# A fused attention, mixture and channel-mixing kernel on one core: buffers that TensorE reads start at multiples of 128 bytes

## Chip, cores and metric

One core of a Trainium2 chip. The metric is the device time of one execution in microseconds (us). The kernel before takes 463.05 us, the median of 3 runs (462.33 to 463.84).

## The reference

Three layers over 2 sequences of 768 tokens with 512 features, all in float32:

```python
# 1. attention, 8 heads of 64: local band (96 back) and 8 global keys, with a slope per head
a = softmax(scale * q @ k.T + bias, masked);  x = a @ v              # (2, 768, 512)
# 2. four causal attention experts, the best two of each token weighted by a gate
logits = x @ w_gate                                                   # (512, 4)
for e in range(4):
    q, k, v = x @ wq[e], x @ wk[e], x @ wv[e]                         # (512, 64) each
    out += weight[e] * (softmax(scale * q @ k.T, causal) @ v @ wo[e])
# 3. token mixing of rank 32, then a channel MLP with a hidden size of 2048
u = out + U/V mixed out
return u + relu(u @ w_ch1) @ w_ch2
```

## The kernel before

**Two forms of a product.** Layer 1 and the attention matrices of layer 2 are plain float32 matmuls. Every product with a weight matrix is made of float32r matmuls: `split_product` (line 1212) takes each operand as a high part and a low part (names ending in h and l) and issues high by high, high by low and low by high into the same PSUM tile. All of its matmuls carry line 1218 in the profile. One operand is the stationary one (loaded by a weight load, 128 columns), the other is the moving one, streamed past it.

```python
for wh, wl, mh, ml in groups:
    for a, m in ((wh, mh), (wh, ml), (wl, mh)):
        last = pe.matmul(dst, a, m, start=start and k == 0, stop=stop and k == n - 1, **kw)
```

**Who uses it.**
- `projected` (line 1274): queries and keys of the experts. Stationary: `wqk_h`, `wqk_l`. Moving: 512 or 256 columns of `xh`, `xl`, the split output of layer 1.
- `values_of` (line 1330): values and gate logits. Stationary: 128 columns of `xh`, `xl`. Moving: a row of 260 columns of `wv_h`, `wv_l` (256 of wv, 4 of w_gate), 12 such matmuls for each of 12 tiles.
- `both_weights` (line 1344): the product of wo and w_ch1, in 8 pieces of 256 columns, 24 matmuls each. Stationary: `woT_h`, `woT_l`. Moving: a piece of w_ch1, which lies in a part of `xh`, `xl` that is free by then (6 pieces), or in `wqk_h`, `wqk_l` (pieces 5 and 6, after the projections are done with them).
- `whole` (line 1558), once for each sequence: u itself. Stationary: `wo_h`, `wo_l`. Moving: the mixed tokens, which lie in `xh[:, 1]`, `xl[:, 1]`.
- `hidden` and `second` (lines 1572 and 1588): the MLP, 32 steps f (16 for each sequence). `hidden(f)` is 12 matmuls, 6 with 512 and 6 with 256 moving columns of `xh`, `xl` against `w01_soon` or `w01_late`. `second(f)` is 24 matmuls, 12 with 512 and 12 with 256 columns of `hidh`, `hidl` against `fh`, `fl`; it reads the same buffers for both sequences.

By these loops there are 720 such matmuls with 512 moving columns (384 in `second`, 192 in `hidden`, 96 in `projected`, 48 in `whole`), 912 with 256 (384, 192, 96, 48, and 192 in `both_weights`) and 144 with 260, 1776 in all.

**The other matmuls.** Transposes (lines 1250, 1383, 1465, 1493) have `prob`, `prob_2`, `o32` as stationary and `ident` as moving operand. Scores (1237, 1449), attention by values (1270, 1482) and the rank product of `nat` by `umix` (1394) are float32 and run in two passes each.

**Order.** Each engine has its own instruction list, written out by hand, with semaphores between them. TensorE's list runs attention with the first projections woven in (from about 0 to 94 us), then the experts' attention with the weight products put between as a filling (list `FILL`, to 238 us), then `whole`, and from 252 us the MLP: `hidden(f+1)` ahead of `second(f)`. In the MLP ScalarE writes `hidh` (line 792), VectorE writes `hidl` (1201) and `fh` (1162), GpSimd writes `fl` (492), and SyncE loads `fraw`. GpSimd also splits the value weights, one row of 260 columns at a time, in `split_weight` (line 504), from `wraw` into `wv_h` and `wv_l`.

**Where buffers begin.** `sb` (line 134) places buffers on each of the 128 partitions one behind the other, each rounded up to 32 bytes. `ident` begins at byte 16512, a multiple of 128. `tie` takes 64 bytes behind it, so what follows begins 64 bytes past a multiple of 128, until `wgt` (192 bytes) ends that; `wv_h` (4 rows of 1040 bytes) and the gate buffers bring it back. For the kernel before this gives:

| begins | buffers that TensorE reads |
|---|---|
| at a multiple of 128 | `ident`, `wqk_h`, `wqk_l`, `wv_h`, `woT_h`, `woT_l`, `wo_h`, `wo_l`, `fh`, `fl`, `w01_soon`, `w01_late`, `mq`, `mk`, `mv`, `prob_2`, `qT`, `kT`, `vN`, `vB` |
| 64 past one | `xh`, `xl`, `prob`, `probT`, `hidh`, `hidl`, `wv_l`, `o32`, `nat`, `umix`, `vmix`, `t3` |

The slices that matmuls take of them begin at further multiples of 128 bytes, but for the value weights: their four rows begin 0, 16, 32 and 48 bytes past a multiple of 128 in `wv_h`, and 64, 80, 96 and 112 in `wv_l`.

Of the kernel before, what the change touches and what calls it, by code (L numbers as in the profile page):

```python
# [15 lines left out]
F32R = mybir.dt.float32r  # L16
# [5 lines left out]
P = 128  # L22
# [6 lines left out]
KT = DM // P  # L29
# [101 lines left out]
def build(nc, t, out):  # L131
    ctx = ExitStack()
    with ctx:
        def sb(name, shape, dt=F32, where=ctx):
            return where.enter_context(nc.sbuf_tensor(name, shape, dt))
# [12 lines left out]

        ident = sb("ident", [P, P])
        tie = sb("tie", [P, E, E])  # L150
        xh = sb("xh", [P, B, KT, S], F32R)
        xl = sb("xl", [P, B, KT, S], F32R)
        prob = sb("prob", [P, 4, S])
# [10 lines left out]
        seps = sb("seps", [P, 2 * (N_UNIT + M_UNIT)])  # L164
        sinv = sb("sinv", [P, 2 * (N_UNIT + M_UNIT)])
        wgt = sb("wgt", [P, 2 * M_UNIT])

        wqk_h = sb("wqk_h", [P, KT, 512], F32R)
        wqk_l = sb("wqk_l", [P, KT, 512], F32R)
        wv_h = sb("wv_h", [P, KT, 260], F32R)  # L170
        wv_l = sb("wv_l", [P, KT, 260], F32R)
        woT_h = sb("woT_h", [P, KT, 2 * P], F32R)
        woT_l = sb("woT_l", [P, KT, 2 * P], F32R)
        wo_h = sb("wo_h", [P, EP, DM], F32R)
# [12 lines left out]
        ginv = sb("ginv", [P, NT])  # L187
        ggt = sb("ggt", [P, NT, E, E])
        geq = sb("geq", [P, NT, E, E])
        o32 = sb("o32", [P, B, EP, S])  # L190
        nat = sb("nat", [P, NT, EP * P])
        umix = sb("umix", [P, NT, 3 * RANK])
# [8 lines left out]
        one, warm = sb("one", [P, 1]), sb("warm", [P, 1])  # L201


        att = ExitStack()
        rel = sb("rel", [P, S], where=att)
        kpos = sb("kpos", [P, 3 * P], where=att)
# [1467 lines left out]
```

## Time and profile before

| what | value |
|---|---|
| median of 3 runs | 463.05 us |
| the profiled execution | 462.32 us |
| its span, first to last instruction | 460.5 us |
| outside the span | 1.8 us |
| instructions | 8488 |
| granted TensorE clock, mean | 0.995 |

A page of the profile gives busy times per engine, the chain of work that ended last, and groups of instructions with the mean duration of one. A matmul's duration there is longer than the distance from its start to the start of the next: they are pipelined, and the duration holds the way through the array too. The chain of waits in order of time counts each instruction only up to the next, so its pieces, divided by their counts, give that distance.

### The profile page before, as it was taken

The numbers are of one execution on the slowest core, as the hardware profiler recorded it, in microseconds if no ns is written. First come the engines' busy times: TensorE is split into PE (matmuls) and PEld (weight loads), VectorE is DVE, ScalarE is ACT, GpSimd is POOL, SyncE is SP. The second block draws the span as 40 slices with busy tenths as digits, with TensorE's granted clock in tenths as the row PEclk, the third lists the DMA queues.
The fourth block names the chain that finished last, engine by engine and source line by source line (L and its number), as shares of the span: only waits on it lengthen the run. The fifth ranks groups of instructions, "written<-read, shape, count | busy, mean of one in ns | idle before, by whom it ended". The sixth has DMA issues, their size and how long they took to land.

```text
span 460.5 us, 8488 instructions
## 1 busy us (share of the span) xinstructions
PE 443.8 (96%) x3194; PEld 369.6 (80%) x3194; DVE 191.3 (42%) x616; ACT 167.3 (36%) x452; POOL 174.1 (38%) x243
## 2 busy tenths in 40 slices
PE   4999999999999999998999999999998999999997
PEld 3677777887787887667998888888887888888886
DVE  4789989455632733655252222222122122222112
ACT  4788788242653654756330111111102101111102
POOL 2667766924961465775112112222221121222210
PEclk9899999999999999999999999999999999999999
DMA  8899950110030011110101011111111033311003
GB/s 246 264 232 290 314 158 1 55 39 2 1 93 0 2 47 48 46 48 1 47 23 47 24 46 47 46 47 30 40 46 47 0 93 91 93 46 47 23 2 137
DMA packets 29949, 33.47 MB, mean 73 GB/s; under 512 B 9204, under 2 KB 19444, under 8 KB 29908
## 3 DMA queue, kind: packets, MB, share of 16 engines
q1 hardware_dynamic: 29474, 32.40, 23.7%
q8 instruction: 26, 0.43, 0.4%
q10 hardware_dynamic: 434, 0.52, 0.3%
q14 instruction: 15, 0.12, 0.1%
HBM read 29.77 MB, written 3.15 MB: 71 GB/s over the span
## 4 chain that ended last, share of the span: by engine, by line
PE 88%; DVE 4%; issue 3%; ACT 2%; DMA 1%; SPq 0%; POOL 0%; DVEq 0%; ACTq 0%
PE ps_s L1218 26%; PE ps_o L1218 25%; PE ps_t L1218 12%; PE ps_s L1449 5%; PE ps_o L1482 4%; PE ps_t L1465 4%; PE ps_o L1270 3%; PE ps_t L1250 3%; PE ps_s L1237 3%; DVE probT L861 1%; PE ps_o L1394 1%; ACT prob L604 1%; DMA kT<-in_k 1%; DVE prob L843 1%; DVE smin L843 0%
## 5 line engine op out<-in xcount | busy, mean ns | idle before, releaser
L492 POOL TENSOR_TENSOR fl<-fraw,fh 128x512 fp32r<-128x512 f32 x32 | 41.4, 1295 | 180.4 <-DVE fh L1162 180.4
L604 ACT ACTIVATE prob<-prob,smin 128x256 f32<-128x256 f32 (+3 forms) x144 | 77.7, 541 | 36.5 <-DVE smin L843 36.1
L792 ACT ACTIVATE hidh<-ps_o 128x768 fp32r<-128x768 f32 x32 | 26.0, 813 | 178.6 <-PE ps_o L1218 178.6
L1201 DVE SCALAR_TENSOR_TENSOR hidl<-ps_o,hidh 128x768 fp32r<-128x768 f32 x32 | 30.7, 958 | 92.8 <-ACT hidh L792 92.8
L541 POOL TENSOR_SCALAR prob<-prob,sinv,one 128x256 f32<-128x256 f32 (+1 forms) x96 | 51.0, 546 | 22.4 <-DVE sinv L874 22.4
L567 POOL TENSOR_SCALAR prob<-prob,sinv,gate 128x128 f32<-128x128 f32 (+5 forms) x48 | 34.5, 728 | 51.7 <-DVE sinv L894 51.6
L1218 PE MATMUL ps_s<-hidl,fh 128*128 128x512 f32 x128 | 50.3, 393 | 0.0
L1218 PE MATMUL ps_s<-hidh,fl 128*128 128x512 f32 x128 | 50.0, 391 | 0.0
L1218 PE MATMUL ps_s<-hidh,fh 128*128 128x512 f32 x128 | 49.9, 390 | 0.0
L1162 DVE CAST fh<-fraw 128x512 fp32r<-128x512 f32 x32 | 14.4, 449 | 69.8 <-PE ps_t L1218 69.8
L1218 PE MATMUL ps_o<-xh,w_late 128*128 128x512 f32 (+1 forms) x160 | 41.9, 334 | 0.0
L843 DVE CUSTOM_DVE_ANT_0 prob<-ps_s,bias 128x256 f32<-128x256 f32 (+1 forms) x96 | 34.5, 398 | 6.7 <-PE ps_s L1237 6.2
L843 DVE CUSTOM_DVE_ANT_0 prob<-ps_s,causal 128x128 f32<-128x128 f32 (+5 forms) x48 | 29.2, 615 | 18.2 <-PE ps_s L1449 11.4
L1218 PE MATMUL ps_t<-hidh,fl 128*128 128x256 f32 x128 | 35.6, 278 | 0.0
L1218 PE MATMUL ps_t<-hidh,fh 128*128 128x256 f32 x128 | 35.5, 278 | 0.0
L1218 PE MATMUL ps_t<-hidl,fh 128*128 128x256 f32 x128 | 35.5, 278 | 0.0
L684 ACT ACTIVATE probT<-ps_t 128x512 f32<-128x512 f32 (+1 forms) x48 | 24.2, 539 | 21.1 <-PE ps_t L1465 21.0
L1218 PEld LDWEIGHTS ps_o<-xh,w_late 128*128 128x128 f32 x160 | 28.6, 188 | 3.3
L1237 PE MATMUL ps_s<-kT,qT 64*128 64x256 f32 (+1 forms) x192 | 27.9, 415 | 3.3 <-DMA kT<-in_k 3.3
L1218 PEld LDWEIGHTS ps_t<-hidh,fh 128*128 128x128 f32 x128 | 24.0, 188 | 5.3
L1218 PEld LDWEIGHTS ps_s<-hidh,fl 128*128 128x128 f32 x128 | 24.0, 188 | 5.1
L1218 PEld LDWEIGHTS ps_t<-hidl,fh 128*128 128x128 f32 x128 | 24.0, 188 | 5.0
(182 smaller groups left out, 980.6 us busy)
## 6 DMA issues: line engine op xcount, KB each, us to landing
fraw<-in_w SPq DMA_DIRECT2D x32, 256.0 KB, 2.7
wraw<-in_w SPq DMA_DIRECT2D x8, 512.0 KB, 3.4
kT<-in_k SPq DMA_DIRECT2D x16, 224.0 KB, 3.9
vN<-in_v SPq DMA_DIRECT2D x8, 384.0 KB, 5.1
out<-prob SPq DMA_DIRECT2D x12, 256.0 KB, 2.7
qT<-in_q SPq DMA_DIRECT2D x7, 384.0 KB, 3.3
vB<-in_v SPq DMA_DIRECT2D x8, 192.0 KB, 5.2
kT<-in_k SPq DMA_DIRECT2D x7, 128.0 KB, 3.5
```

The source lines that it names most:

```text
L492: return pool.tensor_tensor(lo, raw, hi.bitcast(F32), ALU.subtract)
L541: pool.tensor_scalar(x, x, sinv[:, s:s + 1], one[:, 0:1], ALU.mult, ALU.mult).then_inc(norm_done, 1)
L567: pool.tensor_scalar(x, x, sinv[:, col + par:col + par + 1], gate[:, NT * b + i, e:e + 1], ALU.mult, ALU.mult).then_inc(mnorm_done, 1)
L604: act.activation(prob_s, prob_s, ACT.Exp, bias=smin[:, col:col + 1], scale=-1.0, accum_out=ssum[:, col:col + 1]).then_inc(done, 1)
L684: act.activation(flat[:, n0 * P:n1 * P], ps_t[:, g % 2, 0:(n1 - n0) * P], ACT.Copy).then_inc(mevac_done, 1)
L792: act.activation(hidh[:, f % 2, :], ps_o[:, 0:S], ACT.Relu).then_inc(hidh_done, 1)
L843: dve.tensor_tensor_reduce(out=dst, in0=src, in1=mask, scale=-SCALE, scalar=3e38, op0=ALU.add, op1=ALU.min, accum_out=smin[:, col:col + 1] ...
L1201: dve.scalar_tensor_tensor(hidl[:, f % 2, :], ps_o[:, 0:S], 0.0, hidh[:, f % 2, :].bitcast(F32), ALU.max, ALU.subtract).then_inc(hidl_done, 1)
L1218: last = pe.matmul(dst, a, m, start=start and k == 0, stop=stop and k == n - 1, **kw)
L1237: pe.matmul(a_score[s % 8][:, 0:keys.stop - keys.start], qT[half, p % 2, i * P:(i + 1) * P], kT[half, p % 2, keys], start=True, stop=True, ...
L1449: last = pe.matmul(ps_s[:, score_banks(2 * v + par)[0] + k, 0:z - a], mq[half, pp, i * P:(i + 1) * P], mk[half, pp, a:z], start=True, stop ...
L1465: last = pe.transpose(ps_t[:, g % 2, (n - n0) * P:(n - n0 + 1) * P], m_prob[(2 * v + par) % 6][:, j * P:(j + 1) * P], ident[:, :])
```

## The change

Four buffers of 64 bytes that nothing reads or writes are placed ahead of `xh`, `wqk_h`, `o32` and the last group of buffers, and each row of the value weights is 288 columns long in place of 260, of which the first 260 are used as before.

```diff
+        sb("to_xh", [P, 16])
         xh = sb("xh", [P, B, KT, S], F32R)
...
         wgt = sb("wgt", [P, 2 * M_UNIT])
+        sb("to_wqk", [P, 16])
...
-        wv_h = sb("wv_h", [P, KT, 260], F32R)
-        wv_l = sb("wv_l", [P, KT, 260], F32R)
+        wv_h = sb("wv_h", [P, KT, 288], F32R)[:, :, 0:260]
+        wv_l = sb("wv_l", [P, KT, 288], F32R)[:, :, 0:260]
...
         geq = sb("geq", [P, NT, E, E])
+        sb("to_o32", [P, 16])
         o32 = sb("o32", [P, B, EP, S])
...
         one, warm = sb("one", [P, 1]), sb("warm", [P, 1])
+        sb("to_att", [P, 16])
         att = ExitStack()
         rel = sb("rel", [P, S], where=att)
```

By the same placement rule, `xh` then begins at byte 17152 (134 times 128), `wqk_h` at 93440 (730 times 128), `wv_l` at 114432 (894 times 128), `o32` at 148608 (1161 times 128), and the last group at 173824 (1358 times 128). Every buffer of the table above then begins at a multiple of 128, and so does every row of the value weights (1152 bytes, 9 times 128). All buffers together grow by 1152 bytes of a partition.

## Rows read from the trace of the kernel before

**Rows 1.** The page: busy time of TensorE and its weight loads, and its granted clock.
```profile
PE 443.8 (96%) x3194; PEld 369.6 (80%) x3194; DVE 191.3 (42%) x616; ACT 167.3 (36%) x452; POOL 174.1 (38%) x243
...
PEclk9899999999999999999999999999999999999999
```
**Rows 2.** The page: the chain that ended last, by engine and line.
```profile
PE 88%; DVE 4%; issue 3%; ACT 2%; DMA 1%; SPq 0%; POOL 0%; DVEq 0%; ACTq 0%
PE ps_s L1218 26%; PE ps_o L1218 25%; PE ps_t L1218 12%; PE ps_s L1449 5%; PE ps_o L1482 4%; PE ps_t L1465 4%; PE ps_o L1270 3%; PE ps_t L1250 3%; PE ps_s L1237 3%; DVE probT L861 1%; PE ps_o L1394 1%; ACT prob L604 1%; DMA kT<-in_k 1%; DVE prob L843 1%; DVE smin L843 0%
```
**Rows 3.** Busy time in stretches, line 1218 alone (PE, PEld, with counts).
```profile
0.00:460.50 460.50, 295.31 (x1776) 258.84 (x1776) 0.99 0.25 73
```
**Rows 4.** The chain in order of time, MLP, first sequence (start us, us, what).
```profile
294.03 2.05 PE ps_o L1218 x12
296.09 0.69 PE ps_s L1218 x3
296.77 0.34 PE ps_t L1218 x3
...
300.19 2.05 PE ps_o L1218 x12
```
**Rows 5.** The same view, MLP, second sequence.
```profile
403.04 2.08 PE ps_o L1218 x12
405.12 0.69 PE ps_s L1218 x3
405.81 0.35 PE ps_t L1218 x3
...
409.28 0.92 PE ps_o L1218 x4
```
**Rows 6.** The same view, weight products: moving from `xh` (213.76, 226.04), from `wqk_h` (231.38).
```profile
213.76 2.74 PE ps_o L1218 x24
...
226.04 2.75 PE ps_s L1218 x24
228.79 2.59 PE ps_o L1394 x12
231.38 2.85 PE ps_s L1218 x24
```
**Rows 7.** The same view, two value tiles of 12 matmuls each.
```profile
98.51 3.06 PE ps_t L1218 x24
```
**Rows 8.** The same view, transposes: from `prob_2` (194.01), from `prob` (209.62).
```profile
194.01 0.87 PE ps_t L1465 x8
...
209.62 0.88 PE ps_t L1465 x8
```
**Rows 9.** Groups of TensorE by form over the whole span (busy us, mean ns).
```profile
L1218 PE MATMUL ps_s<-hidl,fh 128*128 128x512 f32 x128 | 50.3, 393 | 0.0
L1218 PE MATMUL ps_s<-hidh,fh 128*128 128x512 f32 x128 | 49.9, 390 | 0.0
L1218 PE MATMUL ps_s<-xl,wo_h 128*128 128x512 f32 x16 | 6.3, 395 | 0.0
L1218 PE MATMUL ps_o<-xl,wqk_h 128*128 128x256 f32 x24 | 6.7, 279 | 0.0
L1218 PE MATMUL ps_s<-xh,woT_l 128*128 128x256 f32 x24 | 6.6, 277 | 0.0
L1218 PE MATMUL ps_s<-wqk_l,woT_h 128*128 128x256 f32 x16 | 4.5, 281 | 0.0
L1218 PE MATMUL ps_o<-wv_h,xl 128*128 128x260 f32 x36 | 10.2, 283 | 0.0
L1218 PE MATMUL ps_o<-wv_l,xh 128*128 128x260 f32 x36 | 10.2, 283 | 0.0
```
**Rows 10.** Groups by form, 251 to 350 us (first sequence of the MLP).
```profile
L1218 PE MATMUL ps_t<-hidh,fh 128*128 128x256 f32 x64 | 17.7, 276 | 0.0
```
**Rows 11.** Groups by form, 357 to 455 us (second sequence of the MLP).
```profile
L1218 PE MATMUL ps_t<-hidh,fh 128*128 128x256 f32 x62 | 17.3, 279 | 0.0
```

## The prediction

> **What bounds the kernel now.** I read the page first. TensorE is busy for 443.8 of 460.5 us, every other engine for at most 42% of the span, and the granted clock is at the upper of its two levels (2.4 GHz) in nearly every slice [rows 1]. The chain that ended last lies on TensorE for 88%, and line 1218, the split products, has 26 + 25 + 12 = 63% of it [rows 2]. So nothing has to be uncovered before a faster or slower matmul counts: what a split product gains or loses is gained or lost by the kernel, matmul for matmul. There are 1776 of them [rows 3], 720 with 512 moving columns, 912 with 256, 144 with 260.
>
> The busy time of that line, 295.31 us [rows 3], is close to its share of the chain, but the durations in the groups overlap, so I take the distance from start to start out of the chain in order of time. Three matmuls with 512 columns take 0.69 us, 229 to 230 ns each [rows 4, 5]. Three with 256 columns take 0.34 us in the first sequence and 0.35 in the second [rows 4, 5]. The whole `hidden` tile, 6 of each, takes 2.05 and 2.08 us: with 6 times 229 taken off, one with 256 columns is 113 ns in the first sequence and 118 in the second. The groups say the same by their durations, 276 against 279 ns [rows 10, 11].
>
> **What the change does, part by part.** It adds no instruction, no wait and no transfer, and moves no step. It changes addresses. The semaphores, queues and amounts of data stay. Three things could follow.
>
> 1. The four pads. `xh`, `xl`, `hidh`, `hidl`, `prob`, `probT`, `o32`, `nat`, `umix`, `vmix`, `t3` move from 64 past a multiple of 128 bytes onto one. ScalarE, VectorE and GpSimd read and write several of them too. With 42% busy at most [rows 1], their part costs nothing even if it moved by some per cent: TensorE's unbroken stream in the MLP is the cover, and only in the experts' attention (about 94 to 238 us) would a slower evacuation show. What counts is TensorE.
>
> 2. The rows of the value weights. GpSimd's 4 splits and the 144 matmuls with 260 columns have the same shapes as before. Two tiles of 12 take 3.06 us, 127 ns each with the start of each tile in it [rows 7]. The two kinds of row, 0 to 48 bytes past a multiple of 128 in `wv_h` and 64 to 112 in `wv_l`, have one duration, 283 ns [rows 9]. If the start of a moving row mattered much, these two groups should differ. They don't, so I take 0 for this part. Its bound is what 144 would gain at the low level of the 256-column matmul, 278 in place of 283 ns with the 4 columns more: 0.7 us.
>
> 3. The 1632 other split products. Today their moving operand is 64 past a multiple of 128, except for the 48 with w_ch1 in `wqk_h`, `wqk_l`. Those 48 have both operands on multiples of 128, which is what the change gives to all. They are the nearest row. The tile at 231.38 takes 2.85 us for 24 matmuls; the same tile with its moving operand in `xh` takes 2.74 and 2.75 [rows 6]; by duration 281 against 277 ns [rows 9]. So the one place that already looks like the changed kernel is no faster, if anything 4 to 5 ns slower. For the stationary side the nearest rows are the transposes: from `prob_2` (on a multiple) 8 take 0.87 us, from `prob` (64 past) 0.88 [rows 8]. That is 109 ns either way. I take 0 for both sides. 48 matmuls in one stretch of 6 us are few, so I don't carry their 4 to 5 ns over to all; it is the upper bound.
>
> The time of one 256-column matmul is not fixed by its own addresses alone. `second` reads the same buffers in both sequences, and takes 113 ns in one and 118 in the other [rows 4, 5, 10, 11]. So there are two levels, on which a long stretch settles. A change of addresses can throw that dice again: from one level to the other the 16 steps of a sequence gain or lose 16 times 18 matmuls times 4.5 ns = 1.3 us.
>
> Sum: 462.32 (the profiled execution) + 0 + 0 + 0 = 462.3. This execution lies 0.7 us under the median of the runs shown, so I set the forecast between the two, at 462.7.
>
> A measurement of this kernel tells about 0.3% from no change, 1.4 us. Over 1776 matmuls that is only 0.8 ns each, so "no change" needs the addresses to be nearly without effect.
>
> **Rival A, slower: the relation of the two operands costs.** What TensorE reads at the same time are a moving operand and the next weights. Today they start 64 bytes apart (modulo 128) in nearly all split products; after the change always 0 apart. The 48 that already are 0 apart are the slow ones [rows 6, 9]. Price: 456 matmuls with 256 columns at the low level (288 in the MLP of the first sequence, 24 in its `whole`, 144 weight products) go from about 114.4 to 118.8 ns, 2.0 us. 408 at the high level go from 117.7 to 118.8, 0.4 us. The 720 with 512 columns have no such row; they lie between 0 and the 5 ns by which the worst group of that size stands over the others (395 against 390 to 393 [rows 9]), so 0 to 3.4 us. Together 2.4 to 5.8 us, in the middle 4.1: 466.4. It decides the sign from 0.8 ns a matmul on. For it: the only aligned rows. Against: they are few, and the transposes show no relation. Chance 0.25.
>
> **Rival B, faster by a little: only the high level goes.** Were 64 past a multiple what lets a stretch settle on the high level, the second sequence would run like the first. That is 1.3 us in `hidden` and `second`. The 96 projections with 256 columns (279 against 276 ns [rows 9, 10]) give 0.3, the value rows 0.7, and the 48 weight products 48 times 4.4 ns = 0.2. `whole` has 24 of them in the second sequence, 0.1. Together 2.6 us: 459.7. For it: the two levels exist. Against: the first sequence sits on the low one with the same addresses. Chance 0.22.
>
> **Rival C, faster by much: the excess over the clock goes.** 512 columns at 2.4 GHz are 213.3 ns; the chain shows 229 [rows 4, 5]. The rank product, a float32 stream in two passes, takes 2.59 us for 12 [rows 6], 215.8 ns each against the 213.3 of 512 cycles, so its excess is only 2.5 ns. It too starts 64 past a multiple, but it takes in a column only every second cycle. If a start 64 past a multiple makes a stream at full rate lose one cycle in sixteen, aligned streams lose none. The 720 then gain 13.2 ns each, 9.5 us: 452.8. The far end adds the smaller ones down to the 109 ns of the transposes [rows 8]: 456 times 4.4, 408 times 8.7 and 144 times 9 ns, 6.9 us more, 446. Against it: the 48 aligned ones lose nothing less than the others, and the value rows show no difference. Chance 0.15.
>
> On this point the Trainium skill gives a figure ("TensorE: Matmul & The Clock Gate", the section on the gap of 56 ns): back-to-back warm matmuls with 512 columns start 215.7 ns apart. The trace's 229 differs from it, and the measurement decides what these matmuls cost today. By the page 720 times 13.3 ns, an estimate of 9.6 us, would be there for whoever removes the cause. The page does not say that a start address is the cause. A second page speaks against the change. "SBUF — State Buffer" (Specifications) gives lines of 16 bytes, and every start in the table of buffers is a multiple of 16 already. By that rule no line more is read before than after, and the sum stays at 462.3, as it does by the rows of the value weights.
>
> **How the numbers follow.** No change beyond 0.3%: 0.38. Rivals A, B and C: 0.25, 0.22, 0.15. The forecast is the likeliest case, 462.7. Faster by over 0.3% is B and C, 0.37; slower is A, 0.25. For 8 in 10 the range reaches over B and the smaller half of C down to 454.5, and over A up to 467.0; what is left out is the larger half of C (below 454.5, about 0.09) and the upper end of A with the 512-column term in full (about 0.09).
>
> **What would show it.** In the profile of the changed kernel the instruction counts should be the same, 3194 matmuls and 3194 weight loads. In the chain in order of time, three `ps_s` matmuls of the MLP at 0.69 us and three `ps_t` at 0.34 or 0.35 say no change. 0.70 to 0.71 and 0.36 say rival A. 0.34 in both sequences says B. 0.65 says C. The two weight-product tiles with `wqk_h` as the moving operand keep a relation of 0 modulo 128, so they should stay at 2.85 us; if they change as well, the start modulo 128 is not what sets them, and my nearest row was none. The forecast is wrong if the durations of the 512-column groups leave 390 to 393 ns, or if any engine but TensorE grows in the chain beyond its 4% [rows 2].

## The result, and the profile after

The changed kernel takes 466.25 us (median of 6 runs, 464.37 to 467.53). The kernel before, measured beside it, takes 462.69 (6 runs, 461.73 to 464.15). The ratio is 1.0073, with a 95% interval of 1.0049 to 1.0098: 3.6 us slower. The forecast was 462.7, no change; rival A, slower, has come in, inside the range.

The page of the changed kernel, its busy time and chain:

```profile
span 462.6 us, 8488 instructions
...
PE 446.5 (97%) x3194; PEld 371.4 (80%) x3194; DVE 190.6 (41%) x616; ACT 167.3 (36%) x452; POOL 173.2 (37%) x243
...
PE 88%; DVE 4%; issue 3%; ACT 2%; DMA 1%; SPq 0%; POOL 0%; DVEq 0%; ACTq 0%
```

The same instructions, the same shares of the chain [rows 1, 2]. TensorE alone has more busy time, 446.5 against 443.8 us. The busy time of the split products (line 1223 now), in the view by stretches:

```profile
0.00:463.00 463.00, 299.42 (x1776) 261.85 (x1776) 1.00 0.24 72
```

That is 4.1 us more than before [rows 3], with the same 1776 matmuls. The chain in order of time (start us, us, what), MLP, first sequence and then second:

```profile
300.51 2.10 PE ps_o L1223 x12
302.61 0.70 PE ps_s L1223 x3
303.30 0.36 PE ps_t L1223 x3
...
306.81 0.23 PE ps_o L1223
```

```profile
404.81 2.10 PE ps_o L1223 x12
406.91 0.69 PE ps_s L1223 x3
407.60 0.36 PE ps_t L1223 x3
...
411.11 0.93 PE ps_o L1223 x4
```

The distance from one `hidden` to the next, the period of one MLP step, is the number to follow from here on. Before it is 300.19 - 294.03 = 6.16 us in the first sequence [rows 4] and 409.28 - 403.04 = 6.24 in the second [rows 5]. Now it is 306.81 - 300.51 = 6.30 and 411.11 - 404.81 = 6.30. With 16 steps in the first sequence and some 15 whole ones in the second, that makes 2.2 and 0.9 us. The weight products, same view:

```profile
212.32 2.87 PE ps_o L1223 x24
...
224.87 2.87 PE ps_s L1223 x24
227.73 2.59 PE ps_o L1399 x12
230.33 2.87 PE ps_s L1223 x24
```

Those with their moving operand in `xh` go from 2.74 and 2.75 to 2.87 us [rows 6], 0.13 us a tile and some 0.7 us for the six. The one from `wqk_h` goes from 2.85 to 2.87. The rank product between them keeps its 2.59.

Together this is 3.8 us, so nearly the whole difference lies in the stream of products. The first of them starts here:

```profile
78.42 2.75 PE ps_s L1223 x12
```

From there to the end of the span it is 462.6 - 78.4 = 384.2 us. Before, by the same view, this piece starts at 80.23, and 460.5 - 80.2 = 380.3 us are left: 3.9 us more now. The stage ahead of it moves by itself from run to run. It ended at 78.9, 80.8 and 82.8 us in the profiles of three kernels below (lead3, to_wqk, to_xh) which do the same work up to there, lead3 with the very addresses of the kernel before. It hides part of the difference in a pair of profiles (spans 460.5 and 462.6).

### The profile page after: what moved, and what is told of

It reads as the page before. It is cut to its first block, busy times and chain, and to the rows that moved or that the text cites. A ratio compares the mean times of both kernels' runs of the same rounds, so it can differ in the third digit from the quotient of the medians.

```text
span 462.6 us, 8488 instructions
## 1 busy us (share of the span) xinstructions
PE 446.5 (97%) x3194; PEld 371.4 (80%) x3194; DVE 190.6 (41%) x616; ACT 167.3 (36%) x452; POOL 173.2 (37%) x243
## 4 chain that ended last, share of the span: by engine, by line
PE 88%; DVE 4%; issue 3%; ACT 2%; DMA 1%; SPq 0%; POOL 0%; DVEq 0%; ACTq 0%
PE ps_s L1223 27%; PE ps_o L1223 25%; PE ps_t L1223 12%; PE ps_s L1454 5%; PE ps_o L1487 4%; PE ps_t L1470 4%; PE ps_o L1275 3%; PE ps_s L1242 3%; PE ps_t L1255 3%; DVE probT L866 1%; PE ps_o L1399 1%; ACT prob L609 1%; DMA kT<-in_k 1%; DVE prob L848 1%; DVE smin L848 0%
## 5 line engine op out<-in xcount | busy, mean ns | idle before, releaser
L1223 PE MATMUL ps_s<-hidh,fh 128*128 128x512 f32 x128 | 50.9, 398 | 0.0
```

## The experiments

**What the starts are.** For reading them, one number per matmul: the start of its moving operand minus the start of its weights, in bytes, modulo 256 ("the distance" below). In the kernel before it is 64 for the MLP and the projections (192 - 128), 192 for `whole` and for the weight products from `xh` (192 - 0), and 128 for those from `wqk_h` (128 - 0). In the changed kernel it is 0 for all of these. These are worked out from the order and the sizes of the buffers in each kernel. Each kernel's steps and durations below come from one trace of it; the times come from 5 to 12 runs of each edited kernel, the scans from one run.

**scan.** It leaves the computation out: only matmuls, 32 for each pair of starts, with 128 columns of weights, which one pair loads again for each matmul from the same place. The core of it:

```diff
+for i, (n, m, s) in enumerate(CONFIGS):      # columns, moving start, weights' start (bytes)
+    dst = (ps_a, ps_b)[i % 2]
+    for r in range(32):
+        pe.matmul(dst[:, 0:n], sta[:, s // 4:s // 4 + 128], mov[:, m // 4:m // 4 + n], ...)
```

> This kernel leaves the whole computation out. It only streams float32r matmuls, 32 to a combination, over (256 or 512 moving columns) and over where the moving operand and the weights begin, in bytes past a multiple of 128. Theory R (the relation: the distance of the two starts modulo 128 sets the pace): 256 columns take about 120 ns from start to start wherever the distance is 0 (0 with 0, 64 with 64, 32 with 32) and 113 to 118 where it is 64 (64 with 0, 0 with 64); 512 columns differ by a few ns. Theory M (the moving start alone): every combination with the moving start at 0 is slow, at 64 fast, whatever the weights' start. Theory L (no address matters, a stretch falls on a level by chance): no order by either start.

Measured, 32 matmuls to a piece, chain in order of time. With 256 columns, (moving, weights) = (0, 0), (64, 0), (112, 0), (0, 64), (32, 32), (128, 0), (256, 0):

```profile
15.72 3.83 PE ps_a L60 x32
...
30.88 3.63 PE ps_a L60 x32
...
42.17 3.66 PE ps_b L60 x32
...
45.84 3.77 PE ps_a L60 x32
...
194.63 3.83 PE ps_a L60 x32
...
239.33 3.79 PE ps_a L60 x32
243.12 3.83 PE ps_b L60 x32
```

With 512 columns, (0, 0), (64, 0), (0, 64), (128, 0), (256, 0):

```profile
76.11 7.26 PE ps_a L60 x32
...
105.71 7.33 PE ps_a L60 x32
...
135.31 7.46 PE ps_a L60 x32
...
254.63 7.44 PE ps_a L60 x32
262.08 7.28 PE ps_b L60 x32
```

From start to start, over the last 24 of each, so without the first few, in which a stretch settles (worked out from the single matmuls of the trace):

| distance | 0 | 16 | 32 | 48 | 64 | 80 | 96 | 112 | 128 | 192 | 240 |
|---|---|---|---|---|---|---|---|---|---|---|---|
| 256 columns, ns | 120.0 | 118.7 | 116.7 | 118.4 | 113.3 | 120.0 | 120.0 | 113.3 | 118.8 | 117.8 | 117.0 |
| 512 columns, ns | 226.7 | 231.7 | 233.3 | 233.3 | 228.9 | 231.1 | 233.3 | 231.1 | 232.6 | 233.3 | 226.7 |

At distance 64 the table has the pair (64, 0). The pair (96, 32), also at 64, gave 117.8 ns with 256 columns and the same 228.9 with 512:

```profile
198.46 3.77 PE ps_b L60 x32
```

At the other distances that were taken with several pairs (0, 16, 32, 48 and 224) the pairs agree within 0.1 ns. At 64 two values occur with 256 columns. They are the two levels of the prediction; the runs after next take them up.

Both operands at 0, both at 32 and both at 64 give the same (120.0 and 226.7), so it is not where either begins that counts. (128, 0) is unlike (0, 0), and (256, 0) is like it, as are (512, 0) and (1024, 0): the period is 256 bytes, not 128. Theory R stands, with another period; M falls, and so does L as the whole account, since 512 columns repeat within 0.1 ns at each distance that was taken with several pairs. Long stretches with 512 columns are at their best at distance 0 (and 240), those with 256 columns at their worst (as at 80 and 96).

**to_xh, to_wqk, rows260.** One part of the change alone, twice, and one part undone. Against the kernel before:

```diff
+        sb("to_xh", [P, 16])
         xh = sb("xh", [P, B, KT, S], F32R)
```

> Kernel before with the first pad alone: xh, xl, hidh, hidl at 0, the weights wqk, woT, wo, fh, fl, w01 at 64 past a multiple of 128, so the distance is 64 as in the kernel before. Theory R: as the kernel before, 462.7 us within 0.3%, three 256-column matmuls of the MLP in 0.34 to 0.35 us. Theory M: as the changed kernel, about 466 us, three in 0.36 us.

```diff
+        sb("to_wqk", [P, 16])
         wqk_h = sb("wqk_h", [P, KT, 512], F32R)
```

> Kernel before with the second pad alone: xh, xl, hidh, hidl stay at 64 and the weights move to 64, so the distance is 0 and nothing of them is on a multiple of 128. Theory R: as the changed kernel, about 466 us (ratio 1.007), three 256-column matmuls of the MLP in 0.36 us. Theory M: as the kernel before, 462.7 us.

Against the changed kernel:

```diff
-        wv_h = sb("wv_h", [P, KT, 288], F32R)[:, :, 0:260]
-        wv_l = sb("wv_l", [P, KT, 288], F32R)[:, :, 0:260]
+        wv_h = sb("wv_h", [P, KT, 260], F32R)
+        wv_l = sb("wv_l", [P, KT, 260], F32R)
+        sb("for_wv", [P, 224])
```

> Changed kernel with the rows of the value weights back at 260 columns; a buffer of 896 bytes behind them keeps all that follows where it was. Theories R and M alike: the rows are 144 of 1776 matmuls and had 120 ns each in both kernels, so no difference from the changed kernel, about 466 us. If the rows carried the loss, about 463 us.

| kernel | moving, weights (modulo 128) | distance, MLP | us | ratio to before, interval | MLP step, us |
|---|---|---|---|---|---|
| to_xh | 0, 64 | 64 | 462.74 | 1.0013 (0.9983 to 1.0042) | 6.16, then 6.24 |
| to_wqk | 64, 64 | 0 | 467.24 | 1.0124 (1.0086 to 1.0163) | 6.30, 6.30 |
| rows260 | 0, 0 | 0 | 466.57 | 1.0101 (1.0061 to 1.0142) | 6.30 |

The chain of to_xh, first sequence, and of to_wqk, first sequence:

```profile
296.60 2.05 PE ps_o L1219 x12
...
302.76 0.46 PE ps_o L1219 x2
```

```profile
296.57 2.10 PE ps_o L1219 x12
...
302.87 0.23 PE ps_o L1219
```

to_xh moves `xh`, `xl`, `hidh` and `hidl` onto a multiple of 128, the moving operands of all but the value tiles and the 48 from `wqk_h`, `wqk_l`, and its time can't be told from that of before: the weights moved along, the distance stayed 64. to_wqk puts nothing of this on a multiple of 128 and costs no less than the full change (the intervals of the two ratios overlap). So the loss in the MLP is the distance of 0, and the multiples of 128 play no part. rows260 agrees with the changed kernel, though the two were not measured side by side, so no cost of the rows of the value weights shows.

**by128.** Kernel before with 128 bytes ahead of the weights:

```diff
+        sb("to_wqk", [P, 32])
         wqk_h = sb("wqk_h", [P, KT, 512], F32R)
```

> Kernel before with one buffer of 128 bytes ahead of the weights (wqk, woT, wo, fh, fl, w01 move by 128; every start keeps its place modulo 128). Theory R128 (the distance of the two starts counts modulo 128): no change, about 462 us. Theory R256 (it counts modulo 256, as the scan has it: distance 64 gives 228.9 ns for 512 columns, distance 192 gives 233.3): the MLP and the projections go from distance 64 to 192, 672 matmuls with 512 columns times 4.4 ns = 3.0 us more, whole goes from 192 to 64, 0.2 less, and the 312 matmuls with 256 columns of the first sequence may go from 113.3 to 117.8, 0 to 1.4 us: 2.8 to 4.2 us slower, ratio 1.006 to 1.009.

464.82 us (before beside it 461.63), ratio 1.0065 (1.0041 to 1.0089). Every start kept its place modulo 128, and the time did not stay. So the period of 256 holds in the whole kernel too. The MLP step, chain in order of time:

```profile
296.79 2.08 PE ps_o L1219 x12
...
303.04 2.08 PE ps_o L1219 x12
```

It is 6.25 us, where R256 with distance 192 makes the two sequences 6.16 + 18 times 4.4 ns = 6.24 or more. The step alone would not settle it, since the kernel before has 6.24 in its second sequence at distance 64. The kind of matmul does. In the first sequence (251 to 350 us) one group of `hidden`, before and then by128:

```profile
L1218 PE MATMUL ps_o<-xl,w_late 128*128 128x512 f32 x20 | 7.8, 392 | 0.0
L1218 PE MATMUL ps_o<-xl,w_late 128*128 128x256 f32 x20 | 5.5, 276 | 0.0
```

```profile
L1219 PE MATMUL ps_o<-xl,w_late 128*128 128x512 f32 x20 | 7.9, 396 | 0.0
L1219 PE MATMUL ps_o<-xl,w_late 128*128 128x256 f32 x20 | 5.5, 276 | 0.0
```

Here 512 columns got slower and 256 stayed, as the scan has it for 192 on the low level (233.3 against 228.9 ns). At distance 64 no trace shows that pair: where 512 columns of this group are slower, as in the second sequence of before (394 ns), 256 columns are too (279).

**scan2.** Matmuls alone again, this time with the distance as the only number, in two parts:

```diff
+LEVELS = [(lead, [(256, d, 24)]) for d in (64, 192) for lead in LEADS]
+STEP = lambda d5, d2: [(512, d5, 3), (256, d2, 3)] * 6
```

> This kernel leaves the whole computation out. It streams float32r matmuls over the distance of the two starts, in two parts. First, 24 matmuls with 256 columns at distance 64 and at 192 behind leads of different shape. Theory T (two levels, which the phase of the two streams at the start chooses, and which then hold): 113.3 or 117.8 ns by lead, and the same for all 24. Theory N (one pace for each distance): always the same for one distance. Second, the pattern of the MLP (three with 512, three with 256 columns, six times) at every 16th byte of distance up to 240, and with other distances for 512 than for 256. By the first scan (226.7 ns for 512 at 0 and 240, 228.9 at 64; 113.3 for 256 at 64 or 112, 120 at 0) the six take 1040 ns at distance 0, 1027 at 64 on the low level and 1020 with 0 for 512 and 64 for 256, were there no cost of going from one to the other; the changed kernel shows 1048 at distance 0.

First part, distance 64, without a lead; behind two matmuls with 512 columns; behind one with 512 columns (the leads write to ps_c):

```profile
14.84 2.83 PE ps_a L64 x24
17.66 0.24 PE ps_c L64
17.90 2.83 PE ps_b L64 x24
20.73 0.46 PE ps_c L64 x2
21.19 2.72 PE ps_a L64 x24
```

The same 24 matmuls take 2.83 or 2.72 us, 117.8 or 113.3 ns each from start to start. Of 12 leads (one of them empty), 2 gave the low level at distance 64 (two or three matmuls with 512 columns), and 5 gave it at distance 192. Once settled, within the first few matmuls, a level held to the end of its 24. Theory T stands against N: one distance has two levels. Each lead was run once, so that the same lead gives the same level again is not shown here.

Second part, the MLP's pattern, six times three and three. Distance 0, distance 64, and distance 64 behind three matmuls with 256 columns:

```profile
93.49 6.30 PE ps_a L64 x36
...
118.65 6.32 PE ps_a L64 x36
...
257.21 6.20 PE ps_a L64 x36
```

By single matmuls each six takes 1026 to 1066 ns. Distance 0 gives 1048 and 1052 in turn, the changed kernel's number. Distance 64 gives 1053 without a lead and 1027 behind three matmuls with 256 columns. So distance 64 has three levels in this pattern, with the 1040 of the second sequence. Distance 112 gives 1033 or 1034 in each of the five periods of its one stretch. My estimate of 1020 for distance 0 with 512 columns and 64 with 256 missed: 1037 to 1051. The long stretches can't be added up to the pattern: at distance 0 the three matmuls with 512 columns take 234, 235 and 227 ns in it, against 226.7 in a long stretch. `second` of the changed kernel shows the same, 234, 236 and 228 ns in one such group. So a distance of 0, the best for long stretches with 512 columns, is slower for those of the MLP (229 before). The estimate of 1040 for distance 0 in the expectation missed for the same reason.

**wo128, lead3 and both.** Does the lead choose the level in the kernel as well? Against the kernel before:

```diff
+        sb("to_wo", [P, 32])
         wo_h = sb("wo_h", [P, EP, DM], F32R)
         wo_l = sb("wo_l", [P, EP, DM], F32R)
+        sb("from_wo", [P, 32])
```

> Kernel before with 128 bytes ahead of wo_h and 128 behind wo_l: whole goes from distance 192 to 64, nothing else changes its distance. Theory R256: its 48 matmuls with 512 columns go from 232.9 to about 229 ns, 0.2 us; the one stretch in by128 that went this way showed it. Theory T adds: what follows may settle on another level, so the 256-column matmuls of the second sequence may take 113.3 in place of 117.7 ns: 1.3 us. So 460.2 to 461.5 us where the kernel before has 461.7. Not separable in the times if only the first holds, but in the chain in order of time.

```diff
+                    if b and n == 0:
+                        for _ in range(3):
+                            pe.matmul(ps_s[:, 0, 0:256], xh[:, 1, 2, 0:P], xh[:, 1, 2, 0:256], start=True, stop=True,
+                                      skip_group_check=True)
                     w, cols = slice(m * P, (m + 1) * P), PIECES[k]
```

> Kernel before with three matmuls more, 256 columns at distance 0, ahead of the second whole; they write into a tile that the next matmul starts anew, so the result stays. Theory T (the lead chooses the level): the second sequence of the MLP may leave 117.7 ns for 113.3 ns, 1.3 us less for 0.36 us of added matmuls; it may also settle on a third level or stay, and the first sequence stays at 113.3 ns. Theory A (addresses alone set the pace of a stretch): the second sequence stays at 117.7 ns, and the time grows by 0.36 us.

> Both edits of the two runs beside it. Theory T: a third lead into the second sequence, so again 113.3 or 117.7 ns there, and not of need what either edit alone gives. Theory A: the second sequence stays at 117.7 ns; 461.9 us.

("Both" in the table below is this last one, with the two edits together.)

The MLP step in the second sequence, wo128, then lead3:

```profile
404.32 2.09 PE ps_o L1220 x12
406.41 0.70 PE ps_s L1220 x3
407.11 0.35 PE ps_t L1220 x3
...
410.63 2.09 PE ps_o L1220 x12
```

```profile
401.39 2.05 PE ps_o L1218 x12
403.45 0.69 PE ps_s L1218 x3
404.13 0.34 PE ps_t L1218 x3
...
407.55 2.05 PE ps_o L1218 x12
```

| kernel | MLP step, second sequence | us | ratio to before, interval |
|---|---|---|---|
| before | 6.24 | 462.29 | |
| wo128 | 6.31 | 463.03 | 1.0015 (0.9995 to 1.0035) |
| lead3 | 6.16 | 461.45 | 0.9991 (0.9971 to 1.0012) |
| both | 6.16 | 461.71 | 1.0003 (0.9983 to 1.0024) |

The MLP of the second sequence has the same addresses in all four (modulo 256). It runs at 6.16, 6.24 or 6.31 us a step. What differs is what goes before it. That this, and not chance, chose the level is argued from these traces and not shown, since each kernel was traced once; for it speaks that the traces of before and to_xh, which have the same distances, agree in both sequences, and that the first sequence, with nothing changed ahead of it, has the same level in all four. wo128 missed its forecast of 460.2 to 461.5 us: it saved its 0.2 us in `whole` as forecast, and lost 16 times 0.07 = 1.1 us behind it, on a third level that its expectation had not named. lead3 pays for three matmuls,

```profile
349.32 0.62 PE ps_s L1569 x3
```

and gets 16 times 0.08 = 1.3 us back. What of it is left, 0.7 us, is too little for its interval to tell from the kernel before.

## Why the prediction was wrong

**What bounds the kernel** was right. The same chain, 88% on TensorE, and a few ns on 1776 matmuls came out as 4.1 us of product time and 3.6 us of the kernel's.

**Part 1 and part 2** were right. No other engine grew in the chain, and the rows of the value weights cost and gave nothing: 3.08 us for two tiles against 3.06 [rows 7], and rows260 without a difference from the changed kernel that its interval could tell.

```profile
96.69 3.08 PE ps_t L1223 x24
```

**Part 3 failed**, at the words "I take 0 for both sides". The step weighed each side alone, the weights' start by the transposes [rows 8] and the moving start by the 260-column rows. The pair of them is what counts. The transposes have the distances 0 (`prob_2`) and 192 (`prob`) and agree, but they are plain float32 and have 128 moving columns. In the scan float32r with 128 columns takes 111.7 ns at distance 0 and at 64 alike, so agreement at this size says nothing of 256 or 512 columns. The one row that spoke of pairs [rows 6, 9] I did read, and set aside as too few. It was no chance. It sits at distance 128, for which the scan gives 118.8 ns, and the 2.85 us of 24 are just that. My reading of it as one that "already looks like the changed kernel" was wrong in the period: the changed kernel has distance 0 and 120.0 ns, and this tile moved too, from 2.85 to 2.87 us. The prediction had named that very sign, that the nearest row was none if these tiles changed.

The sizes that the step put at 0 came out as 4.1 us. The signs named for it came too: 0.36 us for three matmuls with 256 columns (in turn with 0.35), and groups with 512 outside 390 to 393 ns:

```profile
L1223 PE MATMUL ps_s<-hidh,fh 128*128 128x512 f32 x128 | 50.9, 398 | 0.0
```

**Rival A** had the mechanism and nearly the size. Its 2.4 us for the 256-column matmuls at 118.8 ns: the weight products came out at 119.6 ns, the MLP's at 117.7 to 118.7. Its 512-column term, 0 to 3.4 us with no row to go by, came out as 232.2 ns in `second` and 231.3 in `hidden` (from 229.0), 230 in the projections (as before), and 229 in `whole` (from 233): 3.2 ns on the 384 and 2.3 on the 192, less 4 on the 48, 1.5 us. The rest, near 2.6 us, is the 256-column matmuls. Mid-price 4.1 us, measured 4.1 in product time and 3.6 in the medians. That the middle was hit is in part luck, since the 512-column term was only a span from 0 to 3.4. Chance 0.25 was too low for the only rival with a row of its own behind it. Its period of 128 was wrong; by it by128 would have run like the kernel before.

**The two levels** were rightly seen as a dice of 1.3 us (6.16 against 6.24 a step), though wo128 shows a third (6.31). **Rival B** fell: in to_xh, with the moving operands on multiples of 128, the high level stayed. Three matmuls put ahead, in lead3, were enough for the low one. At distance 0 no stretch of the changed kernel is on the low level. **Rival C** fell. The excess over 213.3 ns is there at every distance, at least 226.7. What the Trainium skill states for it ("TensorE: Matmul & The Clock Gate", 215.7 ns back to back) no float32r stream with weight loads reached here, and the measurement decides. The same page (Part 2, Step-by-step) has it that loading the next weights does not steal read bandwidth from the running matmul. No run here measures that bandwidth, but the scan's pace hangs on how far apart the two operands start, 113.3 against 120.0 ns with the same instructions, which speaks against the two reads being without effect on each other.

**Open.** Why the period is 256 bytes and why the levels are three is not shown. Whether a lead gives the same level each time was not repeated. A distance of 112 gave 1033 ns for the MLP's pattern, between the low level and the next (1027 and 1040); it was run once, and was not tried in the kernel.

## What to carry to other kernels

Where TensorE's stream of float32r matmuls is the bound, look at the start of the moving operand minus the start of the weights, modulo 256 bytes, and not at whether either is aligned. Putting all on one boundary gives distance 0, good for long runs with 512 columns (226.7 ns) and as slow as any distance for 256 (120.0 against 113.3). These are long-stretch figures: where the two sizes alternate every three matmuls, as in this MLP, 512 columns too were slower at distance 0 (232 against 229). A gap of a few ns between two stretches with the same addresses can be a level on which they have settled, here worth up to 0.15 us a step or 2.4 us a sequence. Before crediting an edit with some tenths of a per cent, compare the steady period of the stretch in the chain, not the totals.

## What the runs showed of the hardware

- The pace of float32r matmuls, each with its own weight load, depends on the distance of the two starts, with a period of 256 bytes: 113.3 to 120.0 ns with 256 columns, 226.7 to 234.5 with 512. With 128 columns (111.7) and 384 (173.3) distances 0 and 64 gave the same.
- At distances 64 and 192 it also has levels, 113.3 and 117.8 ns with 256 columns, and which one came differed with the matmuls ahead. At 64 they held for the 16 steps of a sequence, 100 us, in the kernels; at 192 for the 24 matmuls of scan2.
- A start past a multiple of 128 costs nothing by itself: both operands at 32 or both at 64 take the 120.0 and 226.7 ns of both at 0, and in the kernel the MLP's step is the same with the moving operands at 64 (before) and with the weights at 64 (to_xh), 6.16 and 6.24 us.
- Sizes in alternation are not the sum of their long stretches: at distance 0 three with 512 columns and three with 256 take 1048 to 1052 ns, against 3 times 226.7 and 3 times 120.0, 1040.
